# Expert logits of two blocks moved from the matrix engine to VectorE, and ranks taken in two products

## The reference

```python
def _moe2_ref(x, w_gate, w1, w2, capacity):      # 8 experts, capacity 384
    logits = x @ w_gate
    expert_idx = np.argmax(logits, axis=1)
    gate_w = softmax(logits)[arange(N), expert_idx]
    for i in range(N):                            # rank of a token in its expert
        e = expert_idx[i]
        if counts[e] < capacity:
            disp[e, counts[e]] = x[i]; pos[i] = counts[e]; counts[e] += 1; keep[i] = True
    y = relu(disp @ w1) @ w2                      # per expert
    out[i] = gate_w[i] * y[expert_idx[i], pos[i]] # kept tokens, zero for the others
```

## Time and profile before

| | us |
|---|---|
| median of 3 runs (lowest to highest) | 523.66 (523.17 to 523.76) |
| the profiled execution's own time | 523.87 |
| its span, first to last instruction | 522.1 |
| PE busy | 507.9 (97%) |
| DVE busy | 291.0 (56%) |
| ACT busy | 239.8 (46%) |
| POOL busy | 185.3 (35%) |
| mean granted clock of PE | 0.993 |

### The profile page before, as it was taken

One profiled execution on the slowest core, in us unless ns is written; L12 is line 12 of the kernel. 1 busy time (PEld: TensorE's weight loads), 2 busy tenths in 40 slices (PEclk: granted clock), 3 DMA queues, 4 the chain that ended last, 5 costly groups with the idle time before them and its releaser, 6 DMA issues.

```text
span 522.1 us, 8641 instructions
## 1 busy us (share of the span) xinstructions
PE 507.9 (97%) x3153; PEld 428.3 (82%) x3153; DVE 291.0 (56%) x569; ACT 239.8 (46%) x424; POOL 185.3 (35%) x210
## 2 busy tenths in 40 slices
PE   8999999999999999999999999999999999999993
PEld 8898788888888878888887878898888788888882
DVE  6899664454233343223456645674567878648760
ACT  3899643443222222213443333522457867847620
POOL 3887300000000003000000271027236999999942
PEclk9999999999999999999999999999999999999997
DMA  8987899400000002000223352413786996966100
GB/s 259 259 254 231 285 371 325 141 0 0 2 0 1 2 0 83 0 0 8 105 75 89 124 167 82 119 49 117 242 269 211 379 356 216 357 252 218 47 28 32
DMA packets 28300, 75.08 MB, mean 144 GB/s; under 512 B 5455, under 2 KB 5455, under 8 KB 28240
## 3 DMA queue, kind: packets, MB, share of 16 engines
q1 hardware_dynamic: 24240, 67.97, 39.6%
q0 software_dynamic: 4000, 6.32, 3.4%
HBM read 61.12 MB, written 19.96 MB: 155 GB/s over the span
## 4 chain that ended last, share of the span: by engine, by line
PE 90%; DVE 3%; issue 2%; POOL 1%; ACT 1%; DMA 1%; SPq 0%; ACTq 0%; POOLq 0%
PE bank L1297 9%; PE bank L1299 9%; PE bank L1298 9%; PE bank L1341 9%; PE bank L1343 9%; PE bank L1342 9%; PE bank L1310 7%; PE bank L1262 3%; PE bank L1588 3%; PE bank L1312 3%; PE bank L1590 2%; PE bank L1592 2%; PE bank L1591 2%; PE bank L1289 2%; PE bank L1453 2%
## 5 line engine op out<-in xcount | busy, mean ns | idle before, releaser
L551 POOL DMA_INDIRECT dispatched_rows<-rows,slot_idx x12 | 14.1, 1172 | 268.5 <-issue 145.3
L909 DVE SCALAR_TENSOR_TENSOR g<-g,bank 128x512 f32<-128x512 f32 x48 | 33.0, 687 | 107.6 <-ACT g L638 107.6
L368 POOL TENSOR_TENSOR w_lo<-raw,w_hi 128x256 fp32r<-128x256 f32 x100 | 88.8, 924 | 9.5 <-ACT w_hi L352 9.5
L638 ACT ACTIVATE g<-bank 128x512 f32<-128x512 f32 x48 | 28.6, 597 | 132.8 <-PE bank L1299 132.8
L352 ACT ACTIVATE w_hi<-raw 128x1024 fp32r<-128x1024 f32 x80 | 82.7, 1050 | 0.0
L368 DVE TENSOR_TENSOR w_lo<-raw,w_hi 128x1024 fp32r<-128x1024 f32 (+1 forms) x61 | 72.7, 1193 | 10.1 <-ACT w_hi L352 10.0
L1297 PE MATMUL bank<-x_hi,w_hi 128*128 128x512 f32 x192 | 77.0, 401 | 0.0
L1341 PE MATMUL bank<-w_hi,g_hi 128*128 128x512 f32 x192 | 76.0, 396 | 0.0
L1342 PE MATMUL bank<-w_lo,g_hi 128*128 128x512 f32 x192 | 75.8, 395 | 0.0
L1343 PE MATMUL bank<-w_hi,g_lo 128*128 128x512 f32 x192 | 75.8, 395 | 0.0
L1299 PE MATMUL bank<-x_hi,w_lo 128*128 128x512 f32 x192 | 75.6, 394 | 0.0
(11 more groups left out here) (153 smaller groups left out, 895.8 us busy)
## 6 DMA issues: line engine op xcount, KB each, us to landing
raw<-expert_units SPq DMA_DIRECT2D x64, 512.0 KB, 6.6
raw<-dense_units SPq DMA_DIRECT2D x16, 512.0 KB, 6.9
dispatched_rows<-empty SPq DMA_DIRECT2D x26, 257.0 KB, 10.8
slot_rows<-dispatched_rows SPq DMA_DIRECT2D x26, 257.0 KB, 3.1
tile_in<-attention_tiles SPq DMA_DIRECT2D x12, 384.0 KB, 4.2
tile_in<-attention_tiles SPq DMA_DIRECT2D x12, 336.0 KB, 5.2
queries<-attention_tiles SPq DMA_DIRECT2D x12, 256.0 KB, 5.0
mask<-masks SPq DMA_DIRECT2D x1, 288.0 KB, 4.8
```

Of the source, the lines that this page charges most:

```text
L368: last = engine.tensor_tensor(w_lo[u % RING][:, part], raw[u % RING][:, part], w_hi[u % RING][:, part].bitcast(F32), ALU.subtract)
L909: dve.scalar_tensor_tensor(g32[i % 2][:, :], g32[i % 2][:, :], 1.0, h_bank[i % 2][:, :], ALU.add, ALU.mult).then_inc(s_g, 1)
```

## The change

For the first two blocks the logits no longer come from PE. The gate's weights are given once more, each expert's column as a row of 512 numbers repeated in all 128 partitions, and SP loads them in two halves of 1 MB: one after the scratch rows are filled, one when the first block's hidden products are done. DVE multiplies each token row with each of the 8 gate rows and adds up in the same instruction (`row_logits`, 32 for a block, four in each of the steps n = 1 to 8). `choose` moves to n = 9, `ranks` to n = 10, `place` to n = 11. `choose` also forms running sums of the one-hot columns (`hot_before`), so that `ranks` is two products instead of 10, 14 and (last block) 19. The splits of the 14 expert units move from one in each of the steps 34 to 47 to two in each of the steps 41 to 47. `EARLY_COUNT` goes from 10 to 12, `EARLY_TOKENS` from 12 to 14. The last block's logits are taken as before.

```diff
-    EARLY_COUNT, EARLY_TOKENS = 10, 12
+    EARLY_COUNT, EARLY_TOKENS = 12, 14
+    LOGITS_FROM, LOGITS_EACH = 1, 4
+    CHOOSE_AT, RANKS_AT, PLACE_AT = 9, 10, 11
...
-        split_in_step = {u - AHEAD: u for u in range(AHEAD, U0)}
-        lead = STEPS - FT + 2
-        split_in_step.update({lead + m: U0 + m for m in range(LAST_LEAD)})
+        splits_in_step = {u - AHEAD: [u] for u in range(AHEAD, U0)}
+        lead = STEPS - LAST_LEAD // 2
+        splits_in_step.update({lead + m: [U0 + 2 * m, U0 + 2 * m + 1] for m in range(LAST_LEAD // 2)})
...
             sp.wait_ge(s_fill, 16 * (ALL_SLOTS // P))
+            sp.dma_start(gate_rows[1][:, :, :], gate_rows_in[:, HALF_E:, :]).then_inc(s_gate_rows[1], 16)
+            sp.wait_ge(s_H, FT)
+            sp.dma_start(gate_rows[0][:, :, :], gate_rows_in[:, 0:HALF_E, :]).then_inc(s_gate_rows[0], 16)
...
+            def row_logits(b, j, e):
+                if (b, j, e) == (0, 0, 0):
+                    for half in range(2):
+                        dve.wait_ge(s_gate_rows[half], 16)
...
+                link(dve.scalar_tensor_tensor(products[:, :], rows[:, j, 0:DM], 1.0,
+                                              gate_rows[e // HALF_E][:, e % HALF_E, :], ALU.mult, ALU.mult,
+                                              accum_out=logit[:, j, e:e + 1]))
...
             def choose(b):
-                dve.tensor_copy(onehot_bf[:, :, :], onehot[:, :, :]).then_inc(s_hot, 1)
+                if b:
+                    dve.tensor_copy(hot_before[:, 0, :], hot_before[:, TB, :])
+                else:
+                    dve.memset(hot_before[:, 0, :], 0.0)
+                link(dve.tensor_copy(onehot_bf[:, :, :], onehot[:, :, :]))
+                for j in range(TB):
+                    hot = dve.tensor_tensor(hot_before[:, j + 1, :], hot_before[:, j, :], onehot_bf[:, j, :], ALU.add)
+                    if j < TB - 1:
+                        link(hot)
+                hot.then_inc(s_hot, 1)
...
             def hooks(b, n):
...
+                first = (n - LOGITS_FROM) * LOGITS_EACH
+                for x in range(first, first + LOGITS_EACH):
+                    if 0 <= x < TB * E:
+                        row_logits(b, x // E, x % E)
+                if n == CHOOSE_AT:
                     choose(b)
+                if n == PLACE_AT:
                     place(b)
...
             def ranks(b):
                 pe.wait_ge(s_hot, b + 1)
                 if b:
+                    pe.wait_ge(s_slot, b)
+                dst = r_bank[0][:, 0:TB * E]
+                pe.matmul(dst, ones[:, :], hot_before[:, 0:TB, :], start=True, stop=False)
+                last = pe.matmul(dst, before[:, :], onehot_bf[:, :, :], start=False, stop=True)
...
             def count_before_last():
-                pe.wait_ge(s_earlier, NBLK - 1)
+                pe.wait_ge(s_hot, NBLK - 1)
                 pe.wait_ge(s_slot, NBLK - 1)
```

More of the change, by code:

```diff
@@ L161, in build @@
         yT_at = XB[0] + TB * ROWP * 4
+        HALF_E = E // 2
+        gate_rows = [at(f"gate_rows{i}", [P, HALF_E, DM], F32, o)
+                     for i, o in enumerate([yT_at, gx_at + EMPTY_SIZE])]
+        products = at("products", [P, DM], F32, gx_at)
+        assert HALF_E * DM * 4 <= XB[1] - yT_at and EMPTY_SIZE + HALF_E * DM * 4 <= g_at - gx_at and DM <= ROW
         y_at = [yT_at, yT_at + 2 * KT * P * 4, XB[2], XB[2] + 2 * KT * P * 4]
@@ L291, in build @@
         s_hot = sem("s_hot")
+        s_gate_rows = [sem(f"s_gate_rows{i}") for i in range(2)]
         s_rank = sem("s_rank")
@@ L715, in _ @@
                     g_high(i)
-                if i in split_in_step:
-                    split_hi(act, split_in_step[i])
+                for u in splits_in_step.get(i, []):
+                    split_hi(act, u)
                 if i >= FT:
@@ L737, in early_row @@
                    .then_inc(s_early_row[p], 1)
-            for n in range(4):
-                hooks(NBLK - 1, n)
+            copy_rows(NBLK - 1)
+            for j in range(TB):
+                y_high(j)
             early_relu(0, 0)
-            hooks(NBLK - 1, 5)
+            gate_exp(NBLK - 1)
             for i in range(1, PAIRS):
@@ L1049, in hooks @@
                     copy_rows(b)
[L1050 to L1057, removed]
-                    for j in {3: (0, 1), 5: (2, 3)}.get(n, ()):
-                        copy_logitT(b, j)
-                if n == after(b, 5):
+                first = (n - LOGITS_FROM) * LOGITS_EACH
+                for x in range(first, first + LOGITS_EACH):
+                    if 0 <= x < TB * E:
+                        row_logits(b, x // E, x % E)
+                if n == CHOOSE_AT:
                     choose(b)
-                if n == after(b, 7):
+                if n == PLACE_AT:
                     place(b)
@@ L1389, in ranks @@
                 if b:
[L1390 to L1404 removed]
+                    pe.wait_ge(s_slot, b)
+                dst = r_bank[0][:, 0:TB * E]
+                pe.matmul(dst, ones[:, :], hot_before[:, 0:TB, :], start=True, stop=False)
+                last = pe.matmul(dst, before[:, :], onehot_bf[:, :, :], start=False, stop=True)
                 if b == NBLK - 1:
[L1406 removed]
+                    last = pe.matmul(r_bank[0][:, TB * E:TB * E + E], ones[:, :], hot_before[:, TB, :],
+                                     start=True, stop=True)
                 last.then_inc(s_rank, 1)
             def hooks(b, n):
[L1410 to L1420 removed]
+                if n == RANKS_AT:
                     ranks(b)
             def count_before_last():
[L1425 removed]
+                pe.wait_ge(s_hot, NBLK - 1)
                 pe.wait_ge(s_slot, NBLK - 1)
[L1427 removed]
+                pe.matmul(r_bank[0][:, 0:E], ones[:, :], hot_before[:, TB, :], start=True, stop=True)\
+                  .then_inc(s_before_last, 1)
             def early_transposes(p):
@@ L1445, in early_hidden @@
                 elif n == 2:
-                    pe.wait_ge(s_logitTc, NT)
+                    pe.wait_ge(s_logitTc, TB)
                 else:
@@ L1520, in _ @@
             for j in range(TB):
-                row_transposes(last, j)
+                row_transposes(j)
             early_pair(0, 0)
             for j in range(TB):
-                logits(last, j)
+                logits(j)
             early_hidden(0, 2)
             pe.wait_ge(s_early_xlo, EARLY_TILES)
-            token_logits(last)
+            token_logits()
             early_hidden(0, 3)
@@ L1784 @@
     build(nc, (B, H, S, D, M, E, cap, DFF, EFF), ap["attention_tiles"], ap["masks"], unit,
-          ap["gate_weights"], ap["constants"], out)
+          ap["gate_weights"], ap["gate_rows"], ap["constants"], out)
     r = run_bass_kernel_spmd(nc, [arrays], core_ids=[0])
```

131 lines of the change are left out of this document (45 added, 86 removed).

## The result

The changed kernel took **516.35 us** (median of 4, 516.23 to 516.6) against 523.64 for the kernel before beside it (4, 523.17 to 523.76): a ratio of 0.986, with an interval of 0.9848 to 0.9871. The forecast was 517.3, with a range of 514.2 to 520.6; 7.3 us were gained where 6.4 were forecast. The span went from 522.1 to 514.6 us, at a mean granted clock of 0.995.

The account below looks back on a forecast made before the run. PE was taken as the bound, with 90% of the chain and 97% busy. Terms -9.4 + 0.3 + 0.3 + 0.1 + 0.9 + 1.2 + 0.2 = -6.4 us gave 517.3 us, range 514.2 to 520.6.

Parts of the forecast that it names:

- T(18) to T(41): PE's time from the start of step 18 to that of step 41, said to get 9 us shorter.
- What goes from PE: Transposes, logits and rank products of two blocks leave PE's queue in the dense layer: -9.4 us before other terms.
- The product's price: Each DVE logits product with its sum takes 0.82 us, bounds 0.72 and 1.26, so DVE's step stays under PE's.
- rival 3: Reading out the sum costs a whole linked instruction, 0.94 us a product on DVE: 519.3 us, chance 0.20.
- rival 2: The sum halves DVE's rate, 1.26 us a product, making the kernel slower: 539.5 us, chance 0.09.
- The slack: In the dense layer DVE may be 2.68 us late with `g_low` before PE waits.
- The wait after `choose`: Step 41's longer `choose` (3.9 us) behind two splits makes DVE 2.94 us late, so PE waits 0.3 us.
- The count: PE's `count_before_last` at T(45) waits 0.1 us for `slot_idx`, expected at T(43) + 11.22.
- The early rows: PE waits 0.9 us, bounds 0 and 1.7, near the end of step 46 for the early rows to land.
- The copied rows: After step 47 PE waits 1.2 us, bounds 0.6 and 1.8, for DVE's copy of tile 1.
- The last ranks: PE waits 0.5 us for DVE's one-hot work, three products instead of 19 give back 0.3: +0.2 us.
- rival 1: The stalls don't come: early rows in time, copies not late, sums cheap; 514.6 us, chance 0.14.

Follow-up runs that it names:

- the changed kernel again: The changed kernel run once more, unaltered, as base for the follow-up runs: 516.61 us, ratio 0.9861.
- rows_first: Against the changed kernel, DVE copies the last rows before the two splits of step 47 and the second early tile's low part: 515.26 us, ratio 0.9839.
- logits_only: Against the changed kernel, the ranks are those of before (10, 14 and 19 products): 516.67 us, ratio 0.9865.
- one_split: Against the changed kernel, the 14 splits stand one in each of the steps 34 to 47, as before: 521.42 us, ratio 0.9948.
- early13: Against the changed kernel, the early tiles' transposes come one step sooner (EARLY_TOKENS 13, not 14): 523.58 us, ratio 0.9989.
- ranks_only: Against the kernel before, only the new ranks (running sums, two products a block), with the logits still on PE: 524.19 us, ratio 1.0007.

## Why the prediction was right, point by point

Of the signs that the prediction named, T(18) to T(41) and the wait on the copied rows came; the product lies below its mark (0.72 to 0.74 against 0.75 to 0.87), and the waits on `g_low` in step 43 and on the early rows did not come.

**What goes from PE** (-9.4): right, -9.35. The stretch T(18) to T(41) is 9.2 us shorter where 9 was named as the mark.

**The product's price** (0.82, bounds 0.72 and 1.26): it is 0.73, at the lower bound. The line between 256 and 1024 numbers gave 0.69 for the product, and it is 0.691. The reading is the 82 ns row, which starts before the product's row has ended, 0.61 after its start, and so adds 0.01 and not the 0.10 that I took. A step is 2.08 + 2.92 = 5.0 us, or 4.9 by the start of the first product. This is where rival 3 was half right: there are two instructions, as the Trainium skill says in "VectorE: DVE Perf Modes", section "Two Vector instructions with no wait between them". The price that I gave the second, 0.22 as for any small linked one, was not: over eight steps it would have been late enough to show in T(42) to T(44), and it did not.

**The sum at half rate** (rival 2, 539.5): refuted. The trace gives 691 ns for 512 numbers with both inputs in SBUF, against 687 for `gated`, whose second input is PSUM. The rule of the Trainium skill, "Vector Engine (DVE) Microarchitecture Reference", section 7, that this form halves the rate, does not hold in this kernel; the kernel with six products a step shows the same 0.73 in its steps' length.

**The slack** (2.68): right. `gated` was 2.73 late in step 42 and PE did not wait; with five products it was 0.45 later still and PE waited 0.45 us in step 43, and with six PE waited from the step on in which the queue was more than 2.7 late.

**The wait after `choose`** (0.3): did not come. `choose` took 3.72, not 3.9, and with 2.08 + 0.27 + 2.28 + 3.72 - 5.59 = 2.76 late it was at the edge; and the ranks (0.15), which the prediction left out of the slack, made PE itself come later. **The count** (0.1): `slot_idx` at T(43) + 11.15 against 11.22; nothing was waited for. Both sat on the limit, and no wait at all was within the bounds given.

**The early rows** (0.9, bounds 0 and 1.7): the step that failed by size. The load was issued 8.1 us after `slot_idx`, within the 6.5 to 8.9 that I read from before, but in the changed kernel again it landed in 2.7 to 3.0 us and not 3.9 to 4.2, which brought the first tile 0.4 ahead of PE. My price was taken from a load that ran among others: while it was under way (304.8 to 308.9) the DMA engines were busy 0.85 of the time and moved 262 GB/s, and during the same load of the changed kernel again (314.8 to 317.6) 0.67 and 187 GB/s. That the traffic is the reason fits these numbers but was not tested.

**The copied rows** (1.2, bounds 0.6 and 1.8): right, 1.12, and shown by taking it away (`rows_first`). The prediction left out that the second early tile's transposes now stand in step 47; with the wait of before that they fill, this is the 0.24 in the table.

**The last ranks** (+0.2): +0.06. PE waited 0.47 as expected, and the products gave back 0.4 and not 0.3.

**Not foreseen**: +0.19 to the first expert and +0.48 in the experts, which I said would move as a whole. The runs show where 0.3 of it lies. In expert 6 of the changed kernel again, one split is followed by a gap; DVE's timeline of it, and then of `logits_only`:

```profile
471.05 1.28 DVE L373 TENSOR_TENSOR w_lo<-raw,w_hi 128x512 fp32r<-128x512 f32 x1
472.25 0.55 DVE L1161 TENSOR_REDUCE bank<-bank 128x192 f32<-128x384 f32 x1
```

```profile
471.27 0.80 DVE L375 TENSOR_TENSOR w_lo<-raw,w_hi 128x512 fp32r<-128x512 f32 x1
471.99 0.55 DVE L1161 TENSOR_REDUCE bank<-bank 128x192 f32<-128x384 f32 x1
```

The same split is recorded as 1.28 or 0.80 long, and the chain of waits has 1.06 against 0.58 of "issue" behind its start. The kernel before, `logits_only` and the two kernels with more products have the short form (20.05 to 20.07 us for expert 6); the changed kernel in both its profiles, `rows_first`, `one_split`, `early13` and `ranks_only` have the long one (20.37 to 20.40). The new ranks are in kernels of both sorts, though neither kernel with the old ranks has the long form. Similar losses stand elsewhere in `ranks_only` (expert 4, 14.48 instead of 14.2) and with more products (expert 5, 24.13 instead of 23.8). The changed kernel, `rows_first`, `one_split` and `early13` have equally many instructions ahead on DVE, in different order, and the gap at the same place; the kernels with another number have theirs elsewhere or none, save `ranks_only`. So it may go with the number of instructions ahead rather than with what they compute, but no run tests that, and the cause stays open.

**The sum.** -9.35 + 0.14 - 0.25 + 1.36 + 0.06 + 0.19 + 0.48 - 0.12 = -7.5, against -6.4. Three of the small waits that the forecast had added up, 1.3 us together, did not come, and 0.67 us that it had not foreseen did: so part of its closeness is luck. Without the unforeseen part the run would stand at 515.7, nearer to rival 1 (514.6), two of whose three conditions held. The large terms and their order held, the wait that was largest came, and the forecast's own bounds (515.5 to 518.8) held the time.

## What to carry to other kernels

Work can be taken from a full engine onto one with room as long as the other's queue per step is shorter than the step; what has to be reckoned is the lateness that it hands on (so much over, times the steps, less the slack until its result is needed), and beyond that point the price is whole: here eight products more in a block cost 0.6 us, sixteen 10. Bulk work with room in its deadline belongs after such steps and behind what PE waits for: 4.8 of the 7.3 us hang on the splits moved to the end, and 1.3 more came from letting the copies go ahead of the last splits. Before such work is moved to an earlier step, look at when its data are loaded: in `one_split` a load that stood behind another one on SP's queue made PE wait 1.5 us. A wait that is the difference of two close times may as well be nothing, so the time should be worked out for both ends of its bounds. A transfer's time to landing should be read from a row with like traffic around it, where there is one.

## What the runs showed of the hardware

The product with a sum is two records, 691 and 82 ns, and the second costs 0.01 us over a plain link. A stand of PE of 5.1 us cost again as it came back: 2.2 us in the step that followed, at a granted clock of 0.50 and then 0.86. A gap of 0.3 to 0.5 us can appear at a DVE instruction that did not change, in a place that differs between kernels (experts 4, 5 or 6 here); in a kernel tuned to half a per cent that is as much as an edit's worth, as `ranks_only` shows.
